# A fused attention and expert kernel: dense products whose result nobody reads, divisions two heads later, the second group's slots written out

## The reference, cut to what matters

```
B, H, S, D = 2, 8, 576, 64; N = B*S = 1152 tokens, DM = 512
scores = q @ k.T / sqrt(D)                      # per batch and head, 576 x 576
keep the 32 largest of each row; attn = softmax of those; x = attn @ v
x -> (1152, 512)                                # heads side by side
logits = x @ w_gate + modality_bias[modality]   # 8 experts, F = 1024
e = argmax(logits); out = gate * relu(x @ w1[e]) @ w2[e]        # one expert per token
p = domain_probs / sum                          # 4 dense experts, F = 1024
final = sum over e of p[:, e] * (relu(out @ w1b[e]) @ w2b[e])   # every token, every expert
```

## Time and profile before

| what | us |
|---|---|
| median of two runs | 1041.14 |
| profiled execution, its own time | 1041.25 |
| its span | 1039.5 |
| steps up to the first group's slots (step 46) | to 302.3 |
| steps 46 to 71, with slots beside them | 302.3 to 451.3 |
| rest of the steps up to the last logits | 451.3 to 494.0 |
| second group's table and first weights | 494.0 to 524.4 |
| its slots | 524.4 to 628.3 |
| four dense experts and the stores | 628.3 to 1039.5 |

### The profile page before, as it was taken

How to read it: one execution, slowest core, us unless ns; L and a number is a source line. 1 busy time by engine, 2 the same in 40 slices (tenths; PEclk the granted TensorE clock), 3 DMA queues, 4 the chain that set the end, 5 groups by cost and what they waited for, 6 DMA issues and landing times.

```text
span 1039.5 us, 13434 instructions
## 1 busy us (share of the span) xinstructions
PE 949.6 (91%) x4569; PEld 799.4 (77%) x4570; DVE 559.3 (54%) x1104; ACT 339.0 (33%) x724; POOL 280.3 (27%) x231
## 2 busy tenths in 40 slices
PE   4789999898999889998168997999999999999998
PEld 3668888787877666755157777898999899989897
DVE  5997797679769687980455525333322342314121
ACT  3543434333436354542144524122211131203010
POOL 6684645453456474550201013000000000000000
PEclk8755555555559898999589998999999999999999
DMA  9120000000402323252465336002200220000001
GB/s 204 62 81 21 5 16 1 21 1 20 173 21 91 115 89 112 82 193 102 143 253 192 132 111 230 4 1 81 81 1 1 82 81 0 0 0 0 20 20 50
DMA packets 49303, 75.20 MB, mean 72 GB/s; under 512 B 24608, under 2 KB 24608, under 8 KB 49248
## 3 DMA queue, kind: packets, MB, share of 16 engines
q1 hardware_dynamic: 42160, 61.09, 16.9%
q0 software_dynamic: 4080, 13.37, 4.0%
q10 hardware_dynamic: 3008, 0.05, 0.2%
HBM read 63.23 MB, written 11.27 MB: 72 GB/s over the span
## 4 chain that ended last, share of the span: by engine, by line
PE 57%; issue 19%; POOL 14%; DVE 5%; DMA 3%; ACT 1%; ACTq 0%; PEldq 0%; POOLq 0%; SPq 0%; PEld 0%; DVEq 0%
PE bank L1265 15%; PE bank L1266 15%; PE bank L1267 15%; POOL att L592 9%; POOL att L595 4%; PE bank L1319 3%; PE bank L1376 2%; PE bank L1360 2%; PE bank L1260 2%; DMA y_dram<-b_ys 1%; PE bank L1292 1%; DVE w1l L1140 1%; POOL q_raw L552 1%; DMA w_raw<-in_moe_w_dram 1%; DVE w2l L1140 1%
## 5 line engine op out<-in xcount | busy, mean ns | idle before, releaser
L592 POOL TENSOR_SCALAR att<-sc,top 128x576 f32<-128x576 f32 x70 | 120.7, 1724 | 190.9 <-DVE top L999 190.8
L999 DVE MAX8 top<-work 128x8 f32<-128x576 f32 x216 | 152.2, 744 | 0.1
L1319 PEld LDWEIGHTS bank<-v_one,attT 128*128 128x128 f32 (+3 forms) x800 | 132.6, 248 | 22.9 <-issue 13.4
L1319 PE MATMUL bank<-v_one,attT 128*128 128x65 f32 (+3 forms) x800 | 149.6, 345 | 0.2
L1265 PE MATMUL bank<-xT,w1h 128*128 128x384 f32 x384 | 129.7, 338 | 5.3 <-DVE w1l L1140 5.3
L1266 PE MATMUL bank<-xT,w1l 128*128 128x384 f32 x384 | 129.3, 337 | 0.0
L1267 PE MATMUL bank<-xT,w1h 128*128 128x384 f32 x384 | 129.2, 337 | 0.0
L1202 DVE SCALAR_TENSOR_TENSOR hT<-bank,hT 128x384 fp32r<-128x384 f32 x96 | 53.0, 557 | 131.3 <-ACT hT L902 130.8
L1265 PE MATMUL bank<-w2h,hT 128*128 128x512 f32 x288 | 112.2, 390 | 1.2 <-DVE hT L1202 1.2
L1267 PE MATMUL bank<-w2l,hT 128*128 128x512 f32 x288 | 112.2, 390 | 0.0
L1266 PE MATMUL bank<-w2h,hT 128*128 128x512 f32 x288 | 112.2, 389 | 0.0
(11 more groups left out here) (235 smaller groups left out, 1532.1 us busy)
## 6 DMA issues: line engine op xcount, KB each, us to landing
w_raw<-in_moe_w_dram SPq DMA_DIRECT2D x96, 512.0 KB, 5.4
q_raw<-in_q_dram SPq DMA_DIRECT2D x18, 128.0 KB, 2.6
v_one<-in_v_dram POOLq DMA_DIRECT2D x18, 128.0 KB, 5.6
out_dram<-x_tok SPq DMA_DIRECT2D x9, 256.0 KB, 2.0
k_raw<-in_k_dram SPq DMA_DIRECT2D x8, 256.0 KB, 4.8
y_dram<-zero POOLq DMA_DIRECT2D x2, 1024.0 KB, 6.4
y_dram<-b_ys POOLq DMA_DIRECT2D x7, 256.0 KB, 3.1
x_dram<-x_cur SPq DMA_DIRECT2D x6, 256.0 KB, 2.0
```

The costliest lines, as they stand in the source:

```text
L592: nc.gpsimd.tensor_scalar(att[:, g % ATR, :], sc[:, g % RING, :], top8[:, g % RING, 3, 7:8], None, ALU.is_ge).then_inc(keep_made, 1)
L999: nxt = nc.vector.max(out=top8[:, g % RING, i + 1, :], in_=work[:, j, :])
L1319: last = nc.tensor.matmul(bank[r0:r1, AVB, 0:W], attT[0:kk, g % 2, c, r0:r1], v_one[b][0:kk, h, c, :], start=(c == 0), stop=(c == KC - 1))
```

## The change

1. In TensorE's steps 8 to 45, except 37, 40 and 44 which have other work beside them, `keep_dense` adds four float32 products of 128 x 128 by 128 x 260 on `v_one`, into a PSUM bank that nobody reads (35 times).
2. `normalise` runs one pair later. `X_LAG` and `L_LAG` grow by 2, the first group's ranks move from step 36 to step 37, and VectorE starts the table one pair later. For the last tile the transposes and logits come right after its last head.
3. The first group's slots come every 7 steps (`A_STEP`), with the second product in two parts; the unused guarded slots are passed together by one branch on every engine.
4. The second group's slots are written out one by one, with waits on constants, two gather buffers, two result buffers in two banks, and no wait of a result store on the next gather. `slots_beyond` nests the slots that may not exist; one branch passes all of them.
5. ScalarE gates the first group's tiles (VectorE did), and TensorE transposes them before slot 0 instead of between slot 0 and slot 1. TensorE passes the guards before it sums the second group's tokens. SyncE no longer waits for `a_h`.

The diff, cut (`...` where lines are left out):

```diff
-        EXP_LAG, TR_LAG, AV_LAG, X_LAG, L_LAG = 2, 5, 6, 15, 16
-        STEPS = (T - 1) * H + L_LAG + 1
-        A_START, A_STEP, SPREAD = 46, 8, 5
+        EXP_LAG, TR_LAG, AV_LAG, X_LAG, L_LAG = 2, 5, 6, 17, 18
+        STEPS = (T - 1) * H + AV_LAG + H + 2
+        A_START, A_STEP, SPREAD = 46, 7, 5
...
+            if p >= HEADS + AV_LAG:
+                return T - 1 if p == HEADS + AV_LAG + lag - X_LAG else None
...
+        def slots_beyond(eng, slots, s, slot, ending):
+            if s == GB.slots:
+                ending(s)
+                return
+            with eng.If(slots > s):
+                slot(s)
+                slots_beyond(eng, slots, s + 1, slot, ending)
+            with eng.Else():
+                ending(s)
...
-            sp.wait_ge(a_h, 2 * GA.slots)
             sp.wait_ge(a_d, GA.slots)
             load_kth(0)
...
             def gather_slot(s):
-                nc.gpsimd.tensor_copy(tok_cur[:, :], GB.tok_i[:, bass.DynSlice(s, 1)]).then_inc(tok_picked, 1)
-                wait_reg(pool, (tok_picked, s + 1))
-                nc.gpsimd.indirect_dma_start(b_xs_raw[:, :], ...).then_inc(slot_loaded, 16)
+                nc.gpsimd.indirect_dma_start(b_xs_raw[:, s % 2, :], ...).then_inc(slot_loaded[s % 2], 16)
             def store_slot(s):
-                wait_reg(pool, (slot_y_copied, s + 1 + BASE))
-                pool.dma_start(y_dram[bass.DynSlice(s * P, P), :], b_ys[:, :]).then_inc(slot_stored, 16)
-                wait_reg(pool, (slot_stored, s * 16 + 16))
-                pool.sem_inc(ys_free, 1)
+                pool.wait_ge(slot_y_copied, s + 1)
+                pool.dma_start(y_dram[s * P:(s + 1) * P, :], b_ys[:, s % 2, :]).then_inc(slot_stored[s % 2], 16)
...
+            for t in range(GA.tiles):
+                act.wait_ge(gathered[t], 16)
+                nc.scalar.activation(x_tok[:, t, :], x_tok[:, t, :], ACT.Copy, scale=GA.gate_w[:, t:t + 1]).then_inc(gated, 1)
+            for t in range(GA.tiles):
+                xT_high_part(t)
             split_high(0, w1_raw, w1h, w1_loaded, w1_high)
...
-                if g0 >= H + 2 and (g0 - H - 2) % H == 0:
-                    between = normalise((g0 - H - 2) // H)
+                if g0 >= H + 4 and (g0 - H - 4) % H == 0:
+                    between = normalise((g0 - H - 4) // H)
...
+            def keep_dense(bk):
+                still = v_one[0][:, 0, 0:KC - 1, :].rearrange("p c w -> p (c w)")
+                for i in range(4):
+                    moving = v_one[0][:, i, 0:KC - 1, :].rearrange("p c w -> p (c w)")
+                    nc.tensor.matmul(bank[:, bk, 0:(KC - 1) * W], still[:, 0:P], moving, start=True, stop=True)
...
+                for p in range(H, A_START):
+                    yield from clock.until(p)
+                    if p == (GA.tiles - 1) * H + L_LAG + 3:
+                        ranks(GA)
+                    elif p == (GA.tiles - 1) * H + L_LAG + 6:
+                        sum_tokens(GA)
+                    elif p == A_START - 2:
+                        a_x(0)
+                    else:
+                        keep_dense(MB + 2 if p < (GA.tiles - 1) * H + L_LAG + 6 else MB)
...
             ranks(GB)
-            sum_tokens(GB)
             clock.now = 1000
             for _ in work_beside:
                 pass
+            sum_tokens(GB)
+            for t in range(GA.tiles):
+                x_transposes(t)
             pe.wait_ge(GB.table_made, 2)
...
             for s in range(GB.tiles):
                 slot(s)
+            slots_beyond(pe, slots, GB.tiles, slot, lambda s: None)
```

More of the change, by code:

```diff
@@ L195, in attention_and_experts @@
         b_hsTl = b_mid.take("b_hsTl", [P, FC, P], F32R)
[L196 removed]
+        b_ys = b_mid.take("b_ys", [P, 2, DM])
         grown = Region(nc, at_x, at_end)
@@ L473, in beside @@
                 yield from clock.until(1000)
[L474 to L483, removed]
+                with sp.If(guarded(sp, GA, SPREAD)):
+                    for s in range(SPREAD, GA.slots):
+                        with sp.If(guarded(sp, GA, s)):
+                            a_load1(s)
+                            a_load2(s)
+                            a_store(s)
+                            sp.sem_inc(passed, 1)
+                        with sp.Else():
+                            for c in range(DC):
+                                sp.sem_inc(aw1_loaded[c], 16)
+                                sp.sem_inc(aw2_loaded[c], 16)
+                            sp.sem_inc(a_stored, 16)
+                with sp.Else():
+                    for s in range(SPREAD, GA.slots):
                         sp.sem_inc(a_stored, 16)
@@ L611, in beside @@
                 yield from clock.until(1000)
-                for s in range(SPREAD, GA.slots):
-                    with pool.If(guarded(pool, GA, s)):
-                        a_gather(s)
-                        pool.sem_inc(passed, 1)
+                with pool.If(guarded(pool, GA, SPREAD)):
+                    for s in range(SPREAD, GA.slots):
+                        with pool.If(guarded(pool, GA, s)):
+                            a_gather(s)
+                            pool.sem_inc(passed, 1)
                 pool.wait_ge(a_stored, 16 * GA.slots)
@@ L777, in beside @@
                     a_copy_hT(s, 1)
-                    yield from clock.until(at + 7)
+                    yield from clock.until(at + 6)
                     if s + 1 < SPREAD:
@@ L883, in _ @@
             ke = act.value_load(GB.table_i[0:1, 1, E:E + 1], min_val=1, max_val=E)
[L884 removed]
+            slot_xT(0)
             split_high(0, w2_raw, w2h, w2_loaded, w2_high)
[L886 to L889 removed]
+            for s in range(GB.tiles):
                 slot(s)
[L891 to L895 removed]
+            slots_beyond(act, slots, GB.tiles, slot, lambda s: None)
+            act.wait_ge(slot_h, slots * 2)
             split_high(ke, w1_raw, w1h, w1_loaded, w1_high)
[L897 removed]
+            act.wait_ge(slot_y, slots)
             split_high(ke, w2_raw, w2h, w2_loaded, w2_high)
@@ L1513, in _ @@
             ke = pe.value_load(GB.table_i[0:1, 1, E:E + 1], min_val=1, max_val=E)
-            slot(0)
-            for t in range(GA.tiles):
-                x_transposes(t)
-            with pe.Fori(1, GB.tiles) as s:
+            for s in range(GB.tiles):
                 slot(s)
-            with pe.Fori(GB.tiles, GB.slots) as s:
-                with pe.If(slots > s):
-                    slot(s)
-            pe.wait_ge(slot_relu, slots * 2 + BASE)
-            pe.wait_ge(slot_hT_split, slots * 2 + BASE)
```

292 lines of the change are left out of this document (141 added, 151 removed).

## The result

The changed kernel takes **991.25 us** (median of two runs, 990.09 and 992.42), the kernel before 1041.14 (1040.91 to 1041.38). The ratio is 0.952, with a 95% interval of 0.947 to 0.957: faster by 4.3 to 5.3%. Forecast were 1008.5 us in a range of 990 to 1027; the measured time is 17 us lower, 1.25 us inside the range's lower end, and outside the 998 to 1019 that the forecast gave its own main case. The profiled execution has a span of 988.3 us against 1039.5. In what follows a measured time is the median of all executions of a kernel, while its ratio leaves out an execution that fell in a slower state, one each in experiments 8 and 9.

What follows compares the result with a forecast made beforehand. TensorE at half its clock was taken to bound the attention steps without slots. From 1041.25 us: last logits 14.5 earlier, first weights 9.8, slot 1 6.4, slots 3, less 1 for the jump, giving 1008.5 us; range 990 to 1027.

Steps and rivals of the forecast that it cites:

- main case: Whole kernel: dense products lift TensorE's clock and gapless steps hold it; 1008.5 us, own range 998 to 1019, chance 0.60.
- rival A: Attention steps: the clock does not rise, or not for most, and dense products are paid in full; about 1123 us, chance 0.07.
- B: Rival on attention steps: the clock rises but falls for two steps more in most tiles; 20 us, 1029, chance 0.11.
- D: Rival towards slot 0: first weights start no earlier, 13 of 16 us fall away; 1021 us, chance 0.08.
- Steps 8 to 31: Attention steps at the higher clock: step 31 comes 10 us earlier; a fall at step 13's wait costs about 4.
- Steps 32 to 45: Where VectorE makes the first group's table: moving logits and ranks costs 6 us, leaving step 46 at 298, 4 us earlier.
- Rival C: Steps to 46: the table's chain does not bind, short waits keep the clock; step 46 16 us earlier, 996 us, chance 0.14.
- The divisions: Divisions two heads later: 14 us gained in steps 46 to 71, nothing in steps 8 to 31, where TensorE covered the wait.
- Steps 46 to 71: Steps beside the first group's slots: 7 us more slot work, 14 less from the divisions, 149.0 to 142 us.
- Step 72 to the logits: Rest to the last logits: 42.7 to 39 us, with 7 us less slot work and 3.5 eaten by waits.
- Towards slot 0: From last logits to slot 0: first weights 8.3 us behind the logits instead of 18.1, gather covered by 4 us; 9.8 us gained.
- Slots: Second group's slots 1 to 6 written out: 13.06 us each, 3 us gained; the jump over unwritten slots costs 1 us.

Runs made afterwards that it cites:

- experiment 8: Changed kernel with the first group's table begun in pair 34, ranks in step 36 and two dense products per block: 980.0 us, ratio 0.935.
- experiment 9: Changed kernel with table in pair 34, ranks in step 36, two dense products per block, GpSimd's subtraction for q's low part one head earlier: 968.4 us.
- experiment 1: Changed kernel with the 35 dense blocks left out, all else kept: 1013.9 us, ratio 0.975.
- experiment 6: Changed kernel with TensorE's ranks in step 35 instead of 37, VectorE's program unchanged: 988.8 us, ratio 0.950.
- experiment 5: Changed kernel with the first group's table one pair later (pair 34), ranks in step 39, summed tokens in step 42: 993.8 us, ratio 0.955.
- experiment 7: Changed kernel with the first group's table begun in pair 34, ranks in step 36, summed tokens in step 42: 984.9 us, ratio 0.945.
- experiment 3: Changed kernel with the divisions two heads earlier again, all else kept: 1019.8 us, ratio 0.980.
- experiment 2: Kernel before with nothing but the dense blocks added, at the same steps: 1032.4 us, ratio 0.993.
- experiment 12: Changed kernel with the first group's slots every 8 steps instead of every 7: 989.0 us, ratio 0.948.
- experiment 4: Changed kernel with two dense products per block instead of four: 982.8 us, ratio 0.944.
- experiment 11: Changed kernel with TensorE's sum of the second group's tokens ahead of the guard again: 997.1 us, ratio 0.956.

## Why the prediction was right, and where its steps were off

The sign was right, and the mechanism of the dense products and that of the divisions too. The range held by 1.25 us, and only by the width that was added for the rivals: my own case had 998 to 1019. One of the signs that I had named for being wrong, a wait on VectorE above 13 us for logits or ranks, came (15.59 us). Marks of 4.81 us rule out rival A, no tile has five slow steps (B), and the first weights did start earlier (D). By the spans the forecast gain was 18.5 us short (32.7 against 51.2), more than all of it before step 72 (20.9 us).

- **Steps 8 to 31, mis-sized.** Forecast 10 us, measured 15.2. The plain step is 4.81 us instead of 4.90, which makes 1.6 of the 5.2 missing (18 x 0.09). The fall of the clock in step 13, which I had at 4 us, cost 1.5 (6.28 us from mark 13 to 14, less 4.81), which makes 2.5. The other products gained 4.9 us where I had 4: between marks 14 and 31 the kernel before takes 100.9 us, 8.2 more than 17 plain steps, the changed one 85.1, 3.3 more. The clock came back within the first block behind the wait, as taken; experiment 1 shows that without the dense products it does not rise.
- **Steps 32 to 45, the step that failed.** I had a loss of 6 us; there is a gain of 4.9. I chained the ranks, as the prediction has it, "behind the turn of q's low part" in step 37. The words on the kernel before say themselves that tiles 4 and 5 take both turns in steps 32 and 40, so step 37 has no turn. In the trace the ranks' products start at 215.55 right behind the transposes, and 17 us behind the logits (199.04 to 216.11), where I had 24 (206 to 230). The logits themselves came 7 us earlier than I said, 5 of them from step 31. What does set this stretch is VectorE: experiment 6 takes 5.8 us of its wait away and gains 3.7, experiments 5 and 7 show the wait moving from logits to ranks and then mostly away. Rival C, "the table's chain does not bind", is the nearest in size (it had step 46 16 us earlier than before and 996 us in all; measured are 20.1 and 991.25) but not in its reason: the chain binds, at a lower price.
- **The divisions.** In steps 46 to 71 they are worth 14.2 us, forecast 14 (experiment 3). But the sentence that in steps 8 to 31 "the same wait was covered by TensorE and is worth nothing" priced the cover of the kernel before. The dense products raise the clock, TensorE no longer covers the wait, and there too it costs 9.1 and 10.5 us (experiments 2 and 3). My sum had the divisions already moved when it priced the dense products, so the total did not suffer from this; the split between the two did.
- **Steps 46 to 71.** 11.8 us gained against 7. With the divisions at 14.2, the closer slots took 2.4 us and not 7; experiment 12 has 3.2 for them from the other side. The 7 us were mis-sized: "0.46 slot more" spreads a slot's work evenly over its steps, but what mark 72 cuts off is one quarter of one first product and its transposes (64 records against 60, and 32 against 24).
- **Step 72 to the logits.** Forecast 3.5, nothing came. It is the other half of the same term: 3 us of slot work moved and not 7, and waits ate that: TensorE is busy for 1.5 us less here (36.06 against 37.52), and the stretch is as long as before (42.8 against 42.7).
- **Towards slot 0.** 8.3 us against 9.8. The weights start 7.6 us behind the logits, as forecast within 1. But the rows' gather, which I had "covered, by 4 us", comes last (481.64).
- **Slots.** 13.12 us each, forecast 13.06. The jump over the unwritten slots, for which I took 1 us, shows nowhere: the dense experts wait the same 5.32 us for `w1l` as before, and what it costs TensorE, if anything, lies in that wait.

## What to carry to other kernels

A wait that an engine at half clock covers is not free: price it again at the clock that the change brings, and expect two edits to be worth more together than apart. When a wait for the second link of a chain is in sight, move both links, or the first wait turns into the second. Work that nobody reads can pay on TensorE, but its amount is to be looked for. Here two products in a step held the clock nearly as well as four and let TensorE run ahead, but brought it back later behind a wait, so that most of the lead was lost again in steps 32 to 36. Four right behind a wait and two or none elsewhere was not tried.

## What the runs showed of the hardware

- **TensorE's clock does not follow its busy time.** Busy for 90.00 of 90.00 us it had 0.50 (experiment 1); with the dense products, busy for 87.15 of 90.00, it had 1.00; with half as many, busy for 53.12 of 56.00, it had 0.97. What fills the time matters. The Trainium skill, "TensorE: Matmul & The Clock Gate" (Part 4, "PE-mode transpose"), says that a transpose does not count as busy in the way a product does; these steps hold five transposing products each, but also plain ones, and no run here separates them.
- **The level also depends on what it was.** The kernel before and experiment 1 have no dense products and do the same kind of steps from 42 to 52 us, TensorE busy for nearly the whole time in both. The kernel before, then experiment 1:

```profile
42.00:52.00 10.00, 9.84 (x70) 8.31 (x70) 10.00 (x21) 6.67 (x17) 7.05 (x7) 1.00 0.39 134
```

```profile
42.00:52.00 10.00, 10.00 (x40) 8.59 (x40) 10.00 (x22) 4.12 (x11) 7.03 (x7) 0.50 0.40 134
```

So attention steps run at either level for 10 us. What the dense products change is that the low level is left: experiment 7 began at 0.50 as well (46 to 56 us) and had 1.00 from 66 to 74.
- **At the low clock the dense products cost in full:** 7.18 us a step with two of them (experiment 8). From 84 to 90 us, behind the wait of step 13, the granted clock was 0.95 with four of them, 0.88 and 0.50 in two kernels with two (experiments 4 and 8). Between marks 32 and 36 it was 0.95 with four and 0.54 in both kernels with two.
- **The gather shares its time with the weights.** Issued at 474.24 beside the weights' transfers, the first rows are turned at 481.64; with the weights starting later (experiment 11), issued at 474.88, they are turned at 479.69. So it is in the other traces: 7.1 to 8.4 us wherever the weights run beside the gather, 4.6 in the kernel before and 5.1 in experiment 2, where they start behind it.
